# Attention on one core: the values of the global keys in four 64 x 64 parts of the array, guard and inverse of the sums ahead of the next step's masked blocks

## The chip, the cores and the metric

The kernel runs on one core of a Trainium2 chip. The metric is the device time of one execution in microseconds. A core has five engines with queues of their own: PE (TensorE, matrix products into the PSUM banks), DVE (VectorE), ACT (ScalarE), POOL (GpSimd) and SP (SyncE, here only for issuing DMAs). They are ordered against each other by semaphores alone.

## What is computed

An attention with 8 heads over 4 batches, with 32 global tokens and 512 local ones, followed by two parts with matmuls (a mix of each token with the one before it, then 8 experts with a gate). Only the attention is touched here:

```python
k_all = np.concatenate([k_g, k_l], axis=2)
v_all = np.concatenate([v_g, v_l], axis=2)
s_g = scale * np.matmul(q_g, k_all.transpose(0, 1, 3, 2))
out_g = np.matmul(sm(s_g), v_all)
s_ll = scale * np.matmul(q_l, k_l.transpose(0, 1, 3, 2))
mask = np.abs(pos[:, None] - pos[None, :]) <= window
s_ll = np.where(mask, s_ll, -1000000000.0)
s_lg = scale * np.matmul(q_l, k_g.transpose(0, 1, 3, 2))
a_l = sm(np.concatenate([s_lg, s_ll], axis=-1))
out_l = np.matmul(a_l, np.concatenate([v_g, v_l], axis=2))
```

`sm` subtracts the maximum, takes the exponential and divides by the sum plus 1e-9. A local token sees the 32 global keys and the local ones at most 32 away.

## The kernel before

The heads of a batch are worked on in two quads of four heads. A quad has five units: four of 128 local tokens each (`j` = 0 to 3) and one of the 32 global tokens (`j` is None). So a batch has `UNITS` = 10 units, the attention 40. Each engine has a `step(b, t)` for each unit, written out by hand, and semaphores keep the engines in step. A unit passes through the stages of a pipeline:

- PE, step t: `scores(t)` (L760 for a local unit, with 64 rows and 64 columns of the array, four parts in use; L774 for the global one, 128 rows and 64 columns) into `ps_s`.
- DVE, step t: `mask_scores(t)`: for each of the four heads one block of 160 columns (L1209: scale, mask, negative maximum) into `neg`. For the global unit one instruction (L1217).
- ACT, step t: `exponentials(t)`: for each head one exponential (L1800), with its sum, into `prob` and `rsum`.
- DVE, step t + 1: `guard_sums(t)` adds the 1e-9 (L1228) and `invert_sums(t)` takes the inverse (L1236).
- POOL, step t + 1: it copies the global keys' share of the probabilities (`edge`, L591) and spreads the inverse over 64 columns a head (`rb`, L602, L600 for the global unit), and then does half of a weight chunk of the next part: rounding (L576) or the rest (`lo` part, L580).
- PE, step t + 1: `turn(t)`: transposes of `prob` (L790, L800, and L794 to L796 for the global unit), of `edge` (L792) and of `rb` (L804), which alone waits for `spread`.
- DVE copies one half of the transposes to `probT` (`copy_turned`, L1244, semaphore `probT_b`), ACT the other (L1810, `probT_a`), both behind their other work of step t + 1.
- PE, step t + 2: `apply(t)`: products with the values, into `ps_o`: first the global keys (L827, values `vz`; for head k only rows 32 k to 32 k + 31 of `vz` are not zero), then the local ones (L836). For the global unit L851 to L858.
- DVE, step t + 2: `write_x(t)` (L1258) multiplies by the turned inverse and writes `xT`.

PE's order in a step is scores(t), apply(t - 2), turn(t - 1). DVE's is masked blocks of t, write_x(t - 2), copy_turned(t - 1), with guard and inverse of t - 1 behind the first and the second masked block. For a step with the global unit they stand ahead of everything:

```python
                last = behind(b, t, 1)
                if last and unit(t)[1] is None:
                    guard_sums(*last)
                    invert_sums(*last)
                mask_scores(b, t, last)
```

In the last batch DVE and ACT also do `first_inputs(t)` in each step: the first inputs of the next part (L1282, L1286 `mix_lo` on DVE, L1823, L1827 on ACT). Behind the attention PE goes on with `keys_part(0, GT, 0)`, which waits for those inputs and for POOL's last weight chunk; the last `apply` stands behind it.

SP loads the queries, keys and values of batch b into the same tiles when batch b - 1 has used them.

Of the kernel before, what the change touches and what calls it, by code (L numbers as in the profile page):

```python
# [34 lines left out]
P = 128  # L35
# [5 lines left out]
QB = P // 2  # L41
HALO = 2 * WIN + QB
KW = HALO + SG
HEADS = 4
# [118 lines left out]
def program(nc, qk_t, qg_t, v_t, v_x, v_z, mu, w_9, w_9t, w_mix, w_e, out, x2_d):  # L163
    with ExitStack() as ctx:
# [574 lines left out]
        def _(pe):  # L739
# [67 lines left out]
            def apply(b, t):  # L807
                i, j = unit(t)
                n = UNITS * b + t
                o = ps_o[:, t % 2, :]  # L810

# [9 lines left out]
                if j is not None:  # L821
                    pe.wait_ge(v_loaded[i][j], 16 * (b + 1))
                    if j == 0:
                        pe.wait_ge(vz_loaded[i], 16 * (b + 1))
                    for pair in range(2):
                        for h in range(2):
                            pe.matmul(o[DH * h:DH * (h + 1), P * pair:P * (pair + 1)], vz[i][:, 2 * pair + h, :],  # L827
                                      pt(HEADS), start=(pair == 0), stop=False)
                    for pair in (1, 0):
                        if pair == 0:  # L830
                            pe.wait_ge(probT_a, n + 1)
                        for blk in range(2):
                            for h in range(2):
                                k = 2 * pair + h
                                v0 = HEADS * DH * blk + DH * k
                                mm = pe.matmul(o[DH * h:DH * (h + 1), P * pair + QB * blk:P * pair + QB * (blk + 1)],  # L836
                                               vw[i][:, j, v0:v0 + DH], pt(k, QB * blk, QB), start=False, stop=(pair == 0 and blk == 1))
                else:
                    pe.wait_ge(vx_loaded[i], 16 * (b + 1))
                    rows = P - WIN  # L840
                    for cs in ((2, 3, 4), (0, 1)):
                        if cs[0] == 0:
                            pe.wait_ge(probT_a, n + 1)
                        for pair in range(2):
                            for c in cs:
                                for h in range(2):
                                    k = 2 * pair + h
                                    od = o[DH * h:DH * (h + 1), SG * pair:SG * (pair + 1)]
                                    v0 = HEADS * DH + DH * k
                                    if c < JT - 1:  # L850
                                        mm = pe.matmul(od, vw[i][:, c, v0:v0 + DH], pt(c, SG * k, SG),  # L851
                                                       start=(c == 2 and pair == 0),
                                                       stop=(c == 1 and pair == 1))
                                    elif c < JT:
                                        mm = pe.matmul(od, vw[i][0:rows, c, v0:v0 + DH], pt(c, SG * k, SG, rows),
                                                       start=False, stop=False)
                                    else:
                                        mm = pe.matmul(od, vx[i][:, DH * k:DH * (k + 1)], pt(c, SG * k, SG, rows),  # L858
                                                       start=False, stop=False)
# [326 lines left out]
        def _(dve):  # L1186
# [7 lines left out]

            def mask_scores(b, t, last):

# [8 lines left out]
                if j is not None:  # L1205
                    m = 0 if j == 0 else 2 if j == JT - 1 else 1
                    for k in range(HEADS):
# [3 lines left out]
                                                 negmax[:, t % 2, k:k + 1]).then_inc(masked, 1)  # L1211
                        if last and k == 0:
                            guard_sums(*last)
                        if last and k == 1:
                            invert_sums(*last)
                else:
# [29 lines left out]
            def write_x(b, t):  # L1246
                i, j = unit(t)
                o, sums = ps_o[:, t % 2, :], probT[:, t % 2, 2 * P:4 * P]
                x = xT[:, 2 * i:2 * i + 2, bass.ds(S * b + 1, SG) if j is None else bass.ds(S * b + 1 + SG + P * j, P)]
                dve.wait_ge(applied, UNITS * b + t + 1)  # L1250
                if j is None:
                    sums = sums[:, 0:P].rearrange("p (a h q) -> p a h q", a=2, h=2)
                    for h in range(2):
                        rows = slice(DH * h, DH * (h + 1))
                        ins = dve.tensor_tensor(x[rows], o[rows, 0:2 * SG].rearrange("p (a q) -> p a q", a=2),
                                                sums[rows, :, h, :], ALU.mult)
                else:
                    ins = dve.tensor_tensor(x, o[:, 0:2 * P].rearrange("p (a q) -> p a q", a=2),  # L1258
                                            sums.rearrange("p (a q) -> p a q", a=2), ALU.mult)
                ins.then_inc(x_written, 1)  # L1260

            def step(b, t):

                last = behind(b, t, 1)
                if last and unit(t)[1] is None:
                    guard_sums(*last)
                    invert_sums(*last)
                mask_scores(b, t, last)
                if behind(b, t, 2):
# [862 lines left out]
```

## Time and profile before

| | |
|---|---|
| median of 3 runs | 622.44 us (621.17 to 623.4) |
| profiled execution | 623.0 us, span 621.2 us |
| granted clock of PE over the span | 0.998 |
| PE busy | 607.2 us, 98% |
| DVE busy | 412.6 us, 66% |
| ACT busy | 321.5 us, 52% |
| POOL busy | 172.5 us, 28% |

The span runs from the first to the last instruction of the profiled execution; the difference to its time lies around it. Busy time counts instructions that work, not waiting. Matmuls are pipelined and their ends are modelled, so a busy PE is not one at its peak. PEld are the loads of the array's stationary operand, which overlap the matmuls. A 32-bit matmul shows as two records. The granted clock is the share of the full 2.4 GHz that PE was given.

### The profile page before, as it was taken

To read this page: it belongs to the slowest core of one execution; us is meant where nothing else is said; L and a number is where in the kernel's file an instruction comes from. 1 tells how busy PE (TensorE), PEld (TensorE's weight loads), DVE (VectorE), ACT (ScalarE), POOL (GpSimd) and SP (SyncE) were. 2 spreads that over 40 slices of the span, in tenths; PEclk is the share of its full clock that TensorE was granted. 3 is DMA by queue.
4 is the path that set the end of the run, shared out by engine and by line. 5 is a ranking of instruction groups with operands and counts; after the bars stand their busy time and mean duration, and the time that the engine had idled before them with its cause. 6 is when DMAs were issued, how large, how long until landed. Compare 5 with 4: busy or idle time off the path is not lost.

```text
span 621.2 us, 14687 instructions
## 1 busy us (share of the span) xinstructions
PE 607.2 (98%) x4483; PEld 504.5 (81%) x4484; DVE 412.6 (66%) x1164; ACT 321.5 (52%) x698; POOL 172.5 (28%) x241
## 2 busy tenths in 40 slices
PE   7989999999999999999999999999999999999996
PEld 6878888888888888889979878788788888888885
DVE  4767779845888797786979958957735335463541
ACT  5767779768516614632544844637526225362531
POOL 4545545600000000000000231285632521544141
PEclk9999999999999999999999999999999999999999
DMA  8987786002120010000004751886933512754000
GB/s 307 377 272 249 268 288 212 18 2 85 57 80 0 1 51 18 0 34 35 0 21 168 247 227 52 285 305 221 328 127 106 213 62 81 256 197 154 17 17 15
DMA packets 32935, 84.66 MB, mean 136 GB/s; under 512 B 4602, under 2 KB 7418, under 8 KB 32896
## 3 DMA queue, kind: packets, MB, share of 16 engines
q1 hardware_dynamic: 26816, 70.03, 32.5%
q0 software_dynamic: 3200, 8.92, 4.1%
q10 hardware_dynamic: 2880, 5.24, 2.6%
q8 instruction: 19, 0.31, 0.2%
q14 instruction: 20, 0.16, 0.1%
HBM read 76.04 MB, written 9.70 MB: 138 GB/s over the span
## 4 chain that ended last, share of the span: by engine, by line
PE 90%; DVE 6%; issue 2%; ACT 1%; POOL 1%; DVEq 0%; ACTq 0%; POOLq 0%
PE banks L889 23%; PE banks L891 23%; PE banks L890 23%; PE banks L760 3%; PE banks L1079 3%; PE banks L827 2%; DVE we_lo L1531 2%; PE banks L836 2%; PE banks L790 2%; PE banks L774 1%; PE banks L804 1%; PE banks L998 1%; PE banks L800 1%; PE banks L851 1%; DVE neg L1209 1%
## 5 line engine op out<-in xcount | busy, mean ns | idle before, releaser
L1498 DVE CUSTOM_DVE_ANT_0 product<-x,xT 128x512 f32<-128x512 f32 x120 | 77.8, 687 | 1.2 <-DMA xT<-in_w 1.2
L1800 ACT ACTIVATE prob<-neg,negmax 128x160 f32<-128x160 f32 (+1 forms) x136 | 59.1, 436 | 29.7 <-DVE negmax L1209 20.1
L1778 DVE TENSOR_SCALAR hid<-banks 128x512 f32<-128x512 f32 x34 | 23.5, 690 | 72.6 <-PE banks L891 71.5
L889 PE MATMUL banks<-we_hi,hid_hi 128*128 (+1 forms) x160 | 66.4, 415 | 1.6 <-DVE hid_lo L1611 1.6
L1910 ACT ACTIVATE k_sum<-banks 128x512 f32<-128x512 f32 (+2 forms) x40 | 21.4, 534 | 89.4 <-PE banks L891 84.7
L889 PE MATMUL banks<-we_hi,xg_hi 128*128 (+1 forms) x160 | 64.6, 404 | 1.3 <-DVE we_lo L1531 1.3
L891 PE MATMUL banks<-we_hi,xg_lo 128*128 (+1 forms) x160 | 62.6, 391 | 0.0
L891 PE MATMUL banks<-we_hi,hid_lo 128*128 (+1 forms) x160 | 62.6, 391 | 0.0
L890 PE MATMUL banks<-we_lo,hid_hi 128*128 (+1 forms) x160 | 62.6, 391 | 0.0
L890 PE MATMUL banks<-we_lo,xg_hi 128*128 (+1 forms) x160 | 62.4, 390 | 0.0
L686 POOL MEMSET xg<- 128x1024 f32 x1 | 1.0, 956 | 219.3 <-ACT k_raw L1903 219.3
L889 PE MATMUL banks<-mix_hi,wk_hi 128*128 128x512 f32 (+2 forms) x160 | 57.4, 358 | 0.2 <-POOL wr_lo L580 0.2
L891 PE MATMUL banks<-mix_hi,wk_lo 128*128 128x512 f32 (+2 forms) x160 | 57.1, 357 | 0.0
L890 PE MATMUL banks<-mix_lo,wk_hi 128*128 128x512 f32 (+2 forms) x160 | 57.1, 357 | 0.0
L1962 ACT ACTIVATE hid_hi<-banks 128x512 fp32r<-128x512 f32 x40 | 24.0, 600 | 60.8 <-PE banks L1079 60.7
L648 POOL TENSOR_TENSOR we_lo<-raw_end,we_hi 128x1024 f32 (+1 forms) x16 | 44.4, 2793 | 39.9 <-ACT we_hi L1890 29.8
L1209 DVE CUSTOM_DVE_ANT_0 neg<-banks,mask 128x160 f32<-128x160 f32 x128 | 37.7, 315 | 26.0 <-PE banks L760 24.7
L889 PE MATMUL banks<-wv_hi,k_hi 128*128 128x512 f32 x136 | 53.9, 396 | 0.0
L891 PE MATMUL banks<-wv_hi,k_lo 128*128 128x512 f32 x136 | 53.0, 390 | 0.0
L890 PE MATMUL banks<-wv_lo,k_hi 128*128 128x512 f32 x136 | 53.0, 389 | 0.0
L1611 DVE TENSOR_TENSOR hid_lo<-banks,hid_hi 128x512 fp32r<-128x512 f32 x40 | 27.6, 689 | 29.8 <-ACT hid_hi L1962 29.8
L1531 DVE TENSOR_TENSOR we_lo<-xT,we_hi 128x1024 f32 (+1 forms) x36 | 45.0, 1279 | 0.0
(295 smaller groups left out, 1465.0 us busy)
## 6 DMA issues: line engine op xcount, KB each, us to landing
xT<-in_w_e SPq DMA_DIRECT2D x36, 512.0 KB, 4.4
raw_end<-in_w_e SPq DMA_DIRECT2D x36, 512.0 KB, 4.9
qk<-in_qk_t SPq DMA_DIRECT2D x32, 448.0 KB, 6.3
vw<-in_v_t SPq DMA_DIRECT2D x32, 256.0 KB, 5.4
w_raw<-in_w_mix ACTq DMA_DIRECT2D x20, 256.0 KB, 4.1
x_rows<-x SPq DMA_DIRECT2D x17, 256.0 KB, 2.0
xT<-in_w SPq DMA_DIRECT2D x8, 256.0 KB, 3.4
vz<-in_v_z SPq DMA_DIRECT2D x8, 128.0 KB, 3.5
```

Of the source, the lines that this page charges most:

```text
L648: return pool.tensor_tensor(we_lo[:, buf, 2 * j:2 * j + 2, :].rearrange("p x a b -> p x (a b)"), raw_part(j).unsqueeze(1), we_hi[:, buf, 2 ...
L889: pe.matmul(dst, left[0], right[0], start=first, stop=False)
L890: pe.matmul(dst, left[0], right[1], start=False, stop=False)
L891: return pe.matmul(dst, left[1], right[0], start=False, stop=last)
L1209: dve.tensor_tensor_reduce(neg[:, KW * k:KW * (k + 1)], s[:, h, KW * pair:KW * (pair + 1)], mask[:, m, :], -SCALE, HUGE, ALU.add, ALU.min, ...
L1498: dve.tensor_tensor_reduce(product[:, k % 2, :], x2[:, t, :], w9(e), 1.0, 0.0, ALU.mult, ALU.add, dot[:, t % 2, e:e + 1]).then_inc(dotted, 1)
L1531: dve.tensor_tensor(we_lo[:, buf, 2 * j:2 * j + 2, :].rearrange("p x a b -> p x (a b)"), raw_part(j).unsqueeze(1), we_hi[:, buf, 2 * j:2 * ...
L1611: dve.tensor_tensor(hid_lo[:, D * h:D * (h + 1)], ps_ht[:, h, :], hid_hi[:, D * h:D * (h + 1)].bitcast(F32), ALU.subtract).then_inc(hid_lo ...
L1778: dve.tensor_scalar(hid[:, D * h:D * (h + 1)], ps_h[:, h, :], 0.0, None, ALU.max).then_inc(hid_ready, 1)
L1800: act.activation(prob[:, t % 2, c], neg[:, c], ACT.Exp, scale=-1.0, bias=negmax[:, t % 2, k:k + 1], accum_out=rsum[:, t % 2, k:k + 1]).the ...
L1910: act.activation(k_sum[:, f % 2, 0:w], ps_k[:, f % 2, 0:w], ACT.Relu).then_inc(k_copied, 1)
L1962: act.activation(hid_hi[:, D * h:D * (h + 1)], ps_ht[:, h, :], ACT.Copy).then_inc(hid_hi_ready, 1)
```

## The change

In `apply`, the products of the global keys' values use only the rows that are not zero for the pair of heads: rows 0 to 63 for the first pair, 64 to 127 for the second. With 64 columns for each head, the four matmuls of a unit lie in four parts of the array. Parts with different rows write to different banks, so the sums of a unit now lie in both banks of `ps_o`, one for each pair, in the half `t % 2`, where they had a bank of their own before. The flags that start and stop the sums follow. One semaphore increment is added behind the waits. In DVE's step, guard and inverse of the unit before stand ahead of the masked blocks in each step, not only in those of the global unit.

```diff
-                o = ps_o[:, t % 2, :]
+                o = ps_o[:, :, P * (t % 2):P * (t % 2 + 1)]
...
+                    pe.sem_inc(stepped, 1)
                     for pair in range(2):
+                        rows = slice(2 * SG * pair, 2 * SG * (pair + 1))
                         for h in range(2):
-                            pe.matmul(o[DH * h:DH * (h + 1), P * pair:P * (pair + 1)], vz[i][:, 2 * pair + h, :],
-                                      pt(HEADS), start=(pair == 0), stop=False)
+                            pe.matmul(o[DH * h:DH * (h + 1), pair, :], vz[i][rows, 2 * pair + h, :], pt(HEADS)[rows],
+                                      start=True, stop=False)
...
-                                mm = pe.matmul(o[DH * h:DH * (h + 1), P * pair + QB * blk:P * pair + QB * (blk + 1)],
-                                               vw[i][:, j, v0:v0 + DH], pt(k, QB * blk, QB), start=False, stop=(pair == 0 and blk == 1))
+                                mm = pe.matmul(o[DH * h:DH * (h + 1), pair, QB * blk:QB * (blk + 1)],
+                                               vw[i][:, j, v0:v0 + DH], pt(k, QB * blk, QB), start=False, stop=(blk == 1))
...
-            def mask_scores(b, t, last):
+            def mask_scores(b, t):
...
-                        if last and k == 0:
-                            guard_sums(*last)
-                        if last and k == 1:
-                            invert_sums(*last)
...
-                    ins = dve.tensor_tensor(x, o[:, 0:2 * P].rearrange("p (a q) -> p a q", a=2),
+                    ins = dve.tensor_tensor(x, o,
                                             sums.rearrange("p (a q) -> p a q", a=2), ALU.mult)
...
                 last = behind(b, t, 1)
-                if last and unit(t)[1] is None:
+                if last:
                     guard_sums(*last)
                     invert_sums(*last)
-                mask_scores(b, t, last)
+                mask_scores(b, t)
```

On DVE, in step 3 of the first batch, the queue of the kernel before reads from its first masked block's maximum on (L1228 is the guard, L1236 the inverse, L1209 a masked block and the reading of its maximum):

```order
L1209 ISA negmax 128x1
L1228 TENSOR_TENSOR rsum<-rsum,eps 128x4 [waits exped]
L1209 ISA neg,negmax<-banks,mask 128x160
L1209 ISA negmax 128x1
L1236 RECIPROCAL rinv<-rsum 128x4 [waits spread,summed]
L1209 ISA neg,negmax<-banks,mask 128x160
L1209 ISA negmax 128x1
```

In the changed kernel the same place reads as follows (L1233 is the inverse, L1210 a masked block):

```order
L1233 RECIPROCAL rinv<-rsum 128x4 [waits spread,summed]
L1210 ISA neg,negmax<-banks,mask 128x160 [waits scored,exped]
L1210 ISA negmax 128x1
L1210 ISA neg,negmax<-banks,mask 128x160
L1210 ISA negmax 128x1
L1210 ISA neg,negmax<-banks,mask 128x160
L1210 ISA negmax 128x1
```

The guard (L1225) stands directly ahead of this piece. Both instructions have moved ahead of the first masked block and of its wait for the scores; nothing else of DVE's order has moved.

On PE the order is that of before, here in the same step (L760 scores, L829 the products in question, L838 those with the local values, L790 the first transpose):

```order
L760 MATMUL banks<-qk 64x160 [waits quad0_qk3_loaded,masked]
L760 MATMUL banks<-qk 64x160 x7
L829 MATMUL banks<-probT,vz 64x128 [waits probT_b,quad0_v1_loaded]
L829 MATMUL banks<-probT,vz 64x128 x3
L838 MATMUL banks<-probT,vw 64x64 x4
L838 MATMUL banks<-probT,vw 64x64 [waits probT_a]
L838 MATMUL banks<-probT,vw 64x64 x3
L790 MATMUL banks<-ident,prob 128x128 [waits probT_b,probT_a,exped]
```

What changes on PE is the number of rows that an instruction uses and the bank that it writes, not its place.

## Rows read from the trace of the kernel before

**Rows 1.** The page: busy time of PE, and the chain that ended last, by engine.

```profile
PE 607.2 (98%) x4483; PEld 504.5 (81%) x4484; DVE 412.6 (66%) x1164; ACT 321.5 (52%) x698; POOL 172.5 (28%) x241
...
PE 90%; DVE 6%; issue 2%; ACT 1%; POOL 1%; DVEq 0%; ACTq 0%; POOLq 0%
```

**Rows 2.** By stretch: length, busy PE, PEld, DVE, ACT, POOL, clock, DMA share, GB/s.

```profile
15.60:30.30 14.70, 14.29 (x259) 11.83 (x258) 10.30 (x56) 10.37 (x41) 7.16 (x15) 1.00 1.05 376
30.30:46.50 16.20, 14.65 (x259) 11.91 (x259) 10.44 (x56) 10.35 (x41) 7.93 (x16) 1.00 0.83 276
...
60.48:74.52 14.04, 14.04 (x259) 11.83 (x258) 10.26 (x56) 10.32 (x41) 7.72 (x15) 1.00 0.82 279
...
102.76:118.00 15.24, 15.24 (x287) 13.17 (x288) 14.66 (x63) 14.38 (x50) 9.17 (x16) 1.00 0.12 43
```

**Rows 3.** Chain of waits from 60 to 76 us: start, length, piece.

```profile
61.78 0.47 PE banks L827 x8
...
63.41 0.22 PE banks L804 x2
63.62 0.70 PE banks L760 x16
...
66.19 0.70 PE banks L760 x16
...
69.16 0.70 PE banks L760 x16
69.86 0.59 PE banks L827 x8
70.45 0.47 PE banks L836 x16
70.92 0.37 PE banks L790 x2
...
71.61 0.27 PE banks L804 x2
71.88 0.70 PE banks L760 x16
```

**Rows 4.** Timeline from 60 to 72 us: start, length, engine, instruction.

```profile
60.02 1.28 POOL L580 TENSOR_TENSOR wv_lo<-w_raw,wv_hi 128x512 fp32r<-128x512 f32 x1
...
60.85 0.19 ACT L1800 ACTIVATION_READ_ACCUMULATOR prob<-neg,negmax 128x1 f32 x1
...
61.07 0.25 DVE L1228 TENSOR_TENSOR rsum<-rsum,eps 128x4 f32<-128x4 f32 x1 [0.21 <-ACT prob L1800]
...
61.35 0.18 DVE L1236 RECIPROCAL rinv<-rsum 128x4 f32<-128x4 f32 x1
...
67.64 0.43 ACT L1800 ACTIVATE prob<-neg,negmax 128x160 f32<-128x160 f32 x1 [0.34 <-DVE negmax L1209]
...
69.21 0.18 ACT L1800 ACTIVATION_READ_ACCUMULATOR prob<-neg,negmax 128x1 f32 x1
...
70.18 0.33 DVE L1209 CUSTOM_DVE_ANT_0 neg<-banks,mask 128x160 f32<-128x160 f32 x1 [0.74 <-PE banks L760]
...
70.61 0.43 ACT L1800 ACTIVATE prob<-neg,negmax 128x160 f32<-128x160 f32 x1 [0.75 <-DVE negmax L1209]
...
70.84 0.29 DVE L1209 CUSTOM_DVE_ANT_0 neg<-banks,mask 128x160 f32<-128x160 f32 x1
...
71.06 0.32 DVE L1209 CUSTOM_DVE_ANT_0 neg<-banks,mask 128x160 f32<-128x160 f32 x1
...
71.64 0.55 DVE L1244 COPY probT<-banks 128x384 f32<-128x384 f32 x1
```

**Rows 5.** Timeline in the last batch: POOL's and DVE's subtraction side by side.

```profile
99.40 1.28 POOL L580 TENSOR_TENSOR wv_lo<-w_raw,wv_hi 128x512 fp32r<-128x512 f32 x1
...
100.16 1.07 DVE L1286 TENSOR_TENSOR mix_lo<-first_raw,mix_hi 128x512 fp32r<-128x512 f32 x1
```

More of the change, by code:

```diff
@@ L847, in apply @@
                                     k = 2 * pair + h
-                                    od = o[DH * h:DH * (h + 1), SG * pair:SG * (pair + 1)]
+                                    od = o[DH * h:DH * (h + 1), pair, 0:SG]
                                     v0 = HEADS * DH + DH * k
@@ L851, in apply @@
                                         mm = pe.matmul(od, vw[i][:, c, v0:v0 + DH], pt(c, SG * k, SG),
-                                                       start=(c == 2 and pair == 0),
-                                                       stop=(c == 1 and pair == 1))
+                                                       start=(c == 2), stop=(c == 1))
                                     elif c < JT:
@@ L1247, in write_x @@
                 i, j = unit(t)
-                o, sums = ps_o[:, t % 2, :], probT[:, t % 2, 2 * P:4 * P]
+                o, sums = ps_o[:, :, P * (t % 2):P * (t % 2 + 1)], probT[:, t % 2, 2 * P:4 * P]
                 x = xT[:, 2 * i:2 * i + 2, bass.ds(S * b + 1, SG) if j is None else bass.ds(S * b + 1 + SG + P * j, P)]
@@ L1254, in write_x @@
                         rows = slice(DH * h, DH * (h + 1))
-                        ins = dve.tensor_tensor(x[rows], o[rows, 0:2 * SG].rearrange("p (a q) -> p a q", a=2),
+                        ins = dve.tensor_tensor(x[rows], o[rows, :, 0:SG],
                                                 sums[rows, :, h, :], ALU.mult)
                 else:
-                    ins = dve.tensor_tensor(x, o[:, 0:2 * P].rearrange("p (a q) -> p a q", a=2),
+                    ins = dve.tensor_tensor(x, o,
                                             sums.rearrange("p (a q) -> p a q", a=2), ALU.mult)
```

## The prediction

> **What bounds the kernel now.** I read the page first. Its busy row has PE at 98% of the span, and the chain that ended last is 90% PE [rows 1]. Busy PE in a modelled profile proves little, so I went on to what PE does and waits for around the change. Everything that the diff touches lies in the attention, the first fifth of the span; behind it stand matmuls that the diff doesn't touch and whose first one waits for the end of the attention, so a microsecond won or lost there moves the end by a microsecond. I therefore cut the attention into stretches of one quad (five steps) with the view of busy time by stretch [rows 2]. The reader is to see two stages. In the second quad of batch 1 PE is busy for all of 14.04 us while DVE has 10.26: PE alone sets the pace. In the last batch DVE and ACT also make the first inputs of the next part: in its second quad DVE has 14.66 of 15.24 us and ACT 14.38. There DVE is full and PE only keeps up. In the second quad of batch 0 the DMA engines are full (share 1.05), and the quad behind it takes 16.20 us with PE busy for 14.65.
>
> Next I read the chain of waits inside one PE-bound quad [rows 3]. A piece lasts from the end of the matmuls before it to its own end, so its length is the price of the group with whatever drain stands in front. Last, the timeline of DVE, ACT and POOL in the same quad [rows 4], for how much room there is beside PE.
>
> **The values of the global keys on PE.** The count stays: 4 instructions, 8 records, for each of the 32 local units. Before, each has 128 rows and 64 columns of the array, so two run side by side. Their group takes 0.47 us behind matmuls of the same shape (L774, 128 x 64) and 0.59 behind the scores L760, which use 64 x 64 parts [rows 3]: a change of shape costs 0.12. The change behind L836 gives a second reading of that price: L790 takes 0.37, where two transposes behind transposes of the same shape (L804) take 0.22, so 0.15. What four parts side by side do is seen in L760: 0.70 us less 0.15 of drain is 0.55 for 16 records of 160 columns, 0.21 ns for each record and column; L827 has 0.47 / (8 x 128) = 0.46 ns. Eight records of 128 columns at the rate of L760 take 0.22 us; I take 0.25, since short groups round up.
>
> Now the shapes. Behind local scores the new L829 needs no drain, but L838 behind it, still 128 x 64, does. The unit behind the global scores L774 gets both. So for three of four local units: 0.59 becomes 0.25, and the next group gains 0.15: **-0.19 us**. For the fourth: 0.47 becomes 0.25 + 0.12, the next gains 0.15: **+0.05**. One quad: -0.57 + 0.05 = -0.52.
>
> By TensorEngine Tiling of the Trainium skill, Key Properties, a change of tiling mode drains the array and a change of tile alone doesn't. The 0.12 and 0.15 above agree with it, and it is what speaks against this change: the added drain takes back most of what the four parts give.
>
> The additional semaphore increment in front and the same three waits cost nothing that I can see: L760 has the same form (an increment behind two waits), and its gap in front is no longer than the drain. Its cover was a drain, which L829 no longer has; without it the cost is bounded by 0.06 us a unit, the order of the shortest handover between engines in these rows, doubled (ACT's last sum ends at 61.04, the guard that waits for it begins at 61.07): 0 to 2 us over 32 units. I take 0, because the three waits are over long before in this stage and L760 still streams, and keep the rest for the range.
>
> The new place of the sums (one bank for each pair) changes nothing in time: DVE reads the same 256 elements per partition, and the next unit's matmuls stand behind the copy that DVE does after this reading.
>
> **Guard and inverse in front.** Embedded, they stretch the distance of masked blocks from 0.22 us (70.84 to 71.06) to 0.33 (half of 70.18 to 70.84), twice, so about 0.2 in all. In front of a step's first masked block they run one behind the other: the step with the global scores already has this form: guard at 61.07, inverse at 61.35, and the next instruction could start at about 61.45, 0.38 in all, or 0.28 when DVE is busy before them [rows 4]. They wait for the last exponential of the unit before, which DVE must await before the first block anyway.
>
> In the PE-bound stage this lies in idle time: exponentials end at 69.39, the first block waits for the scores until 70.18, 0.79 us. What it brings: the inverse, now behind the second block and so some 0.6 us behind the start of the first, ends before that start; POOL's spread starts at least 0.6 us earlier, and L804 no longer waits for it. Today that wait is 0.05 (0.27 against 0.22 [rows 3]) in two steps of five, **-0.10** a quad; with a PE that arrives 0.2 earlier and the old place it would be 0.25 in each, which is why the two edits are to be counted together. PE's sum for a quad: -0.62. (A quad of before is 2.57, 2.97, 2.72 and 2.72 us for the steps with local scores, and 3.06 for the one with global scores, the rest of 14.04.)
>
> **What stands next behind PE.** Three cycles get close. (1) Exponentials: four take 1.75 us (67.64 to 69.39), then 0.03 to the guard, 0.38, and 0.43 from first block to first exponential (70.18 to 70.61): 2.59 us a step. PE's own steps become 2.38, 2.97, 2.48, 2.48 and 3.11 (sum 13.4). Those below 2.59 fall short by 0.21 and 0.11, and the long ones behind give it back, so the average is not bound. (2) DVE's copy of the turned blocks ends at 72.19 (71.64 + 0.55), L827 of the next step starts at 72.58: 0.39 to spare. The change takes about 0.2 (shorter step) and 0.12 (no drain) and gives back 0.2 (blocks undisturbed): 0.3 is left, but less the 0.1 to 0.2 of cycle 1. (3) ACT's copy, behind its exponentials, has 0.3 to spare and loses about the same. I allow 0.1 a quad for waits of this kind: **-0.5** a quad.
>
> **The last batch.** Where DVE is full, PE's gain is worth nothing, and guard and inverse cost 0.28 in place of 0.17: +0.11 in six local steps, +0.7. Against it: POOL's subtraction of the weight chunk ends at 100.68, and the DVE subtraction that begins at 100.16 takes 1.07 us, 0.55 of them behind that end [rows 5]. So DVE was held for 0.5 by an operation that stands behind POOL's spread. With the inverse some 0.6 earlier that overlap goes, here and in two like places (0.1 to 0.5 each), -0.9. By SBUF — State Buffer of the Trainium skill, the summary for kernel authors, an instruction of the vector engine with two SBUF inputs and one of GpSimd that reads SBUF exclude each other; this row agrees. I take -0.2 for the batch, between +0.7 and -1.1.
>
> **The sum.** Batches 1 (second quad) and 2: 3 x -0.5 = -1.5. First quad of batch 1, with PE idle for 1.55 us of it: -0.4. Batch 0, with full DMA engines and only two or three units in its first quad: -0.6. Last batch -0.2. Together -2.7 us. The profiled execution took 623.0 (span 621.2), which would give 620.3; the median of the runs shown is 622.4, so the time predicted is 619.7.
>
> **Rivals.**
> - Hidden (the cycles of DVE and ACT eat the gain). For it: slack of only 0.3 in two of them, DVE full in the last batch. Against: ACT, the fuller of the two, has 10.32 of 14.04 us in the PE-bound quad. It would leave -0.1 a quad in six, and +0.0 to +0.7 in the last batch: about -0.5, 621.9.
> - Slower: the row halves don't overlap. The mechanism is at L829: if the four parts take 0.47 as now, a local unit gains 0.03, one behind L774 gains 0.27, less the 0.10: +0.26 a quad, some +2.0 over the attention, and the last batch's +0.7: 625.1. It decides from a group of about 0.38 us upward (0.26 + 0.09 a quad for the last batch, over four units). Against it stands L760, with halves, banks and order laid out alike.
> - POOL holds the guard. At 61.07 the guard lasts 0.25 to 61.32, just when POOL's subtraction (60.02 + 1.28) ends; embedded it would not meet it. If the same happened twice a quad at 0.26 us, it would undo the gain: 622.4. The lock named on the page above is this rule. Against: the spread that releases POOL comes earlier too, and its subtraction then ends about 2.1 us behind a guard, before the next at 2.4 to 2.6.
>
> **How the numbers follow.** A difference of 0.3% (1.9 us) is about what a measurement can tell here. Forecast 0.60, hidden 0.26, POOL 0.05, slower 0.09. The forecast's own spread runs from -1.6 to -4.5 (no waits, cheaper drains, all three holds gone), so some 0.05 of it falls within 0.3%: faster 0.55, same 0.36, slower 0.09. The range goes from 618.2 to 622.4, which takes in the hidden case and leaves out the slower one and the ends.
>
> **What would show it.** L829 in the chain 0.25 behind local scores, L838 0.6 instead of 0.47, L804 always 0.22; a quad of 13.4 to 13.6 us in place of 14.0; a second quad of the last batch within 0.4 of 15.2. I am wrong if L829 takes 0.4 or more, if waits for the copies appear in front of L829, or if the masked blocks begin 0.2 us and more behind the scores in most steps.

## The result: slower by a quarter of a per cent

| | before | after |
|---|---|---|
| median, 22 runs each | 622.14 us (619.89 to 625.06) | 623.58 us (619.53 to 624.52) |
| ratio to before | | 1.0025 (95% interval 1.0015 to 1.0035) |
| profiled execution | 623.0 us, span 621.2 us | 623.91 us, span 621.9 us |
| granted clock of PE over the span | 0.998 | 0.996 |

The forecast was 619.7 us with a range of 618.2 to 622.4. The time lies above the range and on the other side of before. The page of the changed kernel, busy row and chain by engine, answers to [rows 1]:

```profile
PE 606.8 (98%) x4483; PEld 501.0 (81%) x4484; DVE 415.4 (67%) x1164; ACT 321.8 (52%) x698; POOL 176.4 (28%) x241
...
PE 84%; DVE 7%; issue 3%; ACT 2%; POOLq 1%; DMA 1%; POOL 1%; DVEq 0%; ACTq 0%
```

PE's busy time is the same within 0.4 us and its share of the chain fell from 90% to 84%: more of the end hangs on waits, but the page doesn't say where. So I cut the attention into quads, from the start of one L774 to the start of the next. The view by stretch of the changed kernel (columns as in [rows 2]) for the second quad of batch 0, the first of batch 1, the first of batch 2 and the last:

```profile
15.84:34.67 18.83, 15.44 (x259) 12.36 (x258) 11.32 (x57) 10.82 (x42) 7.97 (x14) 0.91 0.90 321
34.67:49.23 14.56, 14.03 (x259) 11.31 (x258) 10.73 (x56) 9.96 (x39) 7.41 (x15) 1.00 0.84 275
62.83:76.53 13.70, 13.64 (x259) 11.11 (x259) 10.96 (x57) 10.35 (x41) 7.54 (x15) 1.00 0.91 300
104.15:118.57 14.42, 13.99 (x259) 11.27 (x259) 14.06 (x61) 13.20 (x45) 8.09 (x14) 1.00 0.14 40
```

In the third of these rows PE is busy nearly throughout, and the quad is shorter than before; the quads in front of it and behind it are like it (table). The first row has PE idle for 3.4 us and a granted clock of 0.91. The last has DVE at 14.06 of 14.42 us. The table holds the same cut for both kernels, worked out from the starts of L774 in the two traces, in us:

| stretch | before | after | difference | forecast |
|---|---|---|---|---|
| up to the first L774 | 15.58 | 15.84 | +0.3 | |
| batch 0, second quad | 14.76 | 18.83 | +4.1 | |
| batch 1, first quad | 16.16 | 14.56 | -1.6 | |
| these three together | 46.50 | 49.23 | +2.7 | -1.0 |
| batch 1 second, batch 2 both | 13.98, 14.05, 13.98 | 13.60, 13.70, 13.59 | -1.1 | -1.5 |
| batch 3, first and second | 14.25, 13.89 | 14.03, 14.42 | +0.3 | -0.2 |
| attention to the next part's first matmul | 122.18 | 124.14 | +2.0 | -2.7 |

What lies behind the attention took 499.0 us in the profiled execution of before and 497.5 to 498.1 in those of all other kernels of this study, the changed one too. That execution of before was 0.9 above its median, and its surplus lay there, so only the attention is compared from here on.

**The PE-bound quads.** The chain of waits of the changed kernel (start, length, piece) answers to [rows 3]:

```profile
64.13 0.38 PE banks L829 x8
64.50 0.62 PE banks L838 x16
...
65.82 0.22 PE banks L804 x2
...
66.74 0.34 PE banks L829 x8
67.08 0.62 PE banks L838 x16
...
72.11 0.06 issue
72.17 0.45 PE banks L829 x8
...
74.15 0.70 PE banks L760 x16
74.85 0.22 PE banks L829 x8
75.07 0.62 PE banks L838 x16
```

L829 takes 0.22 us behind local scores when nothing holds it (74.85), 0.38 behind L774, and the drain has moved to L838 (0.62). L804 is 0.22 each time. But twice L829 is longer, 0.34 and 0.45. The two PE-bound quads beside this one have two longer pieces each as well, here in batch 1:

```profile
58.39 0.34 PE banks L829 x8
...
60.97 0.31 PE banks L829 x8
61.28 0.70 PE banks L838 x16
```

The timeline shows what holds L829 there. DVE's copy of the turned blocks ends at 58.14, and the first load of L829 begins 0.12 us later:

```profile
57.58 0.56 DVE L1241 COPY probT<-banks 128x384 f32<-128x384 f32 x1
58.26 0.24 PEld L829 LDWEIGHTS banks<-probT,vz 64*64 64x64 f32 x8 [0.16 <-issue]
```

It is 0.12 in all four long pieces of those two quads, so L829 waits for this copy. In the quad shown first it is not so: there the copies end 0.41 and 0.31 us ahead of L829's first load. These are the first local step of the loop's second pass and the first one with the batch's new values; what holds L829 in them is not shown.

**Batch 0.** The timeline of PE in the changed kernel (start, length, line; in brackets the idle time in front and what ended it):

```profile
25.11 0.78 PE L760 MATMUL banks<-qk 64*64 64x160 f32 x16
25.70 0.40 PE L829 MATMUL banks<-probT,vz 64*64 64x128 f32 x6
28.83 0.38 PE L829 MATMUL banks<-probT,vz 64*64 64x128 f32 x2 [2.73 <-issue]
29.14 0.69 PE L838 MATMUL banks<-probT,vw 128*64 128x64 f32 x16
```

PE stops in the middle of a group, behind the sixth of its eight records, where no wait stands in the program, for 2.73 us. Nothing in the profile released it: "issue" is time in which it waited for nothing that the profile shows. The same view of before:

```profile
25.08 0.66 PE L827 MATMUL banks<-probT,vz 128*64 128x128 f32 x8
26.14 0.69 PE L836 MATMUL banks<-probT,vw 128*64 128x64 f32 x16 [0.41 <-issue]
```

The same kind of stop, at nearly the same place, 0.41 us long. The views by stretch up to the stop, of the changed kernel and then of before, give the count of records in front of it: 339 + 341 = 680 and 341 + 342 = 683.

```profile
0.00:28.80 28.80, 22.38 (x339) 17.63 (x341) 15.58 (x87) 17.59 (x67) 13.79 (x35) 1.00 0.96 338
```

```profile
0.00:26.10 26.10, 22.37 (x341) 18.00 (x342) 14.02 (x84) 16.19 (x60) 12.62 (x33) 1.00 0.96 334
```

More stops of this kind, of 0.2 to 0.74 us, stand in before at 19.18, 34.02 and 41.34 us, with 248 and 249 records from one to the next and 237 up to the last, and in the changed kernel at 20.13 and 44.16. A stop at a fixed count of PE's records, with no semaphore behind it, looks like code that has not arrived. The view of the DMA queues bears it out: for 0.25 us from 26.00 in the changed kernel, and from 23.25 in before (packets, MB, share of 16 engines):

```profile
q1 hardware_dynamic: 30, 0.09, 95.5%
q8 instruction: 1, 0.02, 29.7%
```

```profile
q1 hardware_dynamic: 19, 0.06, 60.0%
q10 hardware_dynamic: 19, 0.04, 41.2%
q8 instruction: 1, 0.02, 25.9%
```

One packet of 16 KB on queue q8, kind "instruction", amid data that nearly fill the 16 engines. It starts at 26.05 in the changed kernel and at 23.47 in before, 2.8 and 2.7 us before PE resumes (28.83, 26.14). This distance holds everywhere: from 14 to 62 us the 18 profiles of this study have 29 stops of PE over 0.3 us that nothing released, and each ends 2.3 to 2.8 us after such a packet starts. In the changed kernel the packet starts just as PE comes to its stop (28.83 - 2.73 = 26.10), 2.6 us later than in before, so almost its whole way is paid for.

Whose packets are they? PE runs batch 0 as straight-line code and batches 1 to 3 as three passes of one loop. The packets of q8 come every 4 to 11 us up to the end of the loop's first pass (the last at 61.30 in before, 63.52 in the changed kernel), and none comes in any profile from 67 to 118 us, in the passes that repeat the same code. The view of the queues of before from 66 to 118 us has instruction packets of q14 alone:

```profile
q1 hardware_dynamic: 4375, 8.62, 49.4%
q10 hardware_dynamic: 1296, 2.36, 14.2%
q14 instruction: 5, 0.04, 0.2%
```

The stop has a second price. By stretches of 2 us in the changed kernel (last three columns: granted clock, DMA share, GB/s):

```profile
26.00:28.00 2.00, 0.10 (x3) 0.00 (x0) 1.15 (x9) 1.59 (x8) 0.99 (x3) 1.00 1.04 369
28.00:30.00 2.00, 1.17 (x20) 0.93 (x20) 0.13 (x1) 0.30 (x2) 0.00 (x0) 0.98 1.04 380
30.00:32.00 2.00, 2.00 (x19) 1.63 (x21) 1.10 (x4) 0.58 (x1) 0.82 (x3) 0.50 0.88 307
32.00:34.00 2.00, 2.00 (x38) 1.56 (x31) 1.08 (x9) 0.66 (x4) 1.11 (x1) 0.67 0.19 67
```

Behind a pause of nearly 3 us the granted clock is 0.50 from 30 to 32 us, which is 1.2 GHz, and 0.67 from 32 to 34, a mean of both levels. PE is busy for all of these 4 us and does 0.50 and 0.67 of a stretch's work: 1.0 + 0.66 = 1.7 us lost. Some comes back: the DMA share has fallen to 0.19 by 32 us, PE is idle for 0.53 us in the first quad of batch 1 and not for 1.55, and that quad is 1.6 us shorter than before.

The single profile is no exception. Each execution has its mean granted clock on record: in 19 of the 22 of the changed kernel it is 0.997 or less, and in 3 of 35 of before (those beside runs 1 to 4). But a stop of this length need not cost the clock. Run 3 below has the same stop, 2.46 us long, and stays at 1.00 behind it:

```profile
30.00:32.00 2.00, 2.00 (x46) 1.63 (x44) 1.40 (x7) 0.62 (x2) 1.21 (x3) 1.00 0.92 316
```

### The profile page after: what moved, and what is told of

It reads as the page before. It is cut to its first block, busy times and chain, and to the rows that moved or that the text cites. A ratio compares the mean times of both kernels' runs of the same rounds, so it can differ in the third digit from the quotient of the medians.

```text
span 621.9 us, 14714 instructions
## 1 busy us (share of the span) xinstructions
PE 606.8 (98%) x4483; PEld 501.0 (81%) x4484; DVE 415.4 (67%) x1164; ACT 321.8 (52%) x698; POOL 176.4 (28%) x241
## 4 chain that ended last, share of the span: by engine, by line
PE 84%; DVE 7%; issue 3%; ACT 2%; POOLq 1%; DMA 1%; POOL 1%; DVEq 0%; ACTq 0%
PE banks L890 22%; PE banks L892 22%; PE banks L891 22%; PE banks L760 3%; PE banks L1080 3%; PE banks L838 2%; DVE we_lo L1528 2%; PE banks L790 1%; PE banks L829 1%; PE banks L999 1%; DVE neg L1210 1%; PE banks L774 1%; PE banks L800 1%; POOLq L724 1%; DMA xg<-x_rows,rows_in 1%
## 5 line engine op out<-in xcount | busy, mean ns | idle before, releaser
L1528 DVE TENSOR_TENSOR we_lo<-xT,we_hi 128x1024 f32 (+1 forms) x36 | 42.9, 1220 | 0.0
L1210 DVE CUSTOM_DVE_ANT_0 neg<-banks,mask 128x160 f32<-128x160 f32 x128 | 34.0, 321 | 13.3 <-PE banks L760 11.7
```

What stands on the lines that cost most here:

```text
L1210: dve.tensor_tensor_reduce(neg[:, KW * k:KW * (k + 1)], s[:, h, KW * pair:KW * (pair + 1)], mask[:, m, :], -SCALE, HUGE, ALU.add, ALU.min, ...
L1528: dve.tensor_tensor(we_lo[:, buf, 2 * j:2 * j + 2, :].rearrange("p x a b -> p x (a b)"), raw_part(j).unsqueeze(1), we_hi[:, buf, 2 * j:2 * ...
```

## The experiments

Three theories: **the increments** in PE's straight-line code of batch 0 make its code arrive later among full-length loads; guard and inverse in front cost in **the last batch**; **the four parts** bring less than counted. (The letters in the recorded expectations are their own: in runs 1 to 3 A is the last batch and B the increment with the loads of code, in 5 and 6 C is the length of PE's code.) The attention's length is that of one profiled execution each, which can lie some us off its median.

**1. The four parts alone.** The changed kernel with guard and inverse between the masked blocks, as before:

```diff
...
-                if last:
+                if last and unit(t)[1] is None:
```

> The four parts alone; guard and inverse stay between the masked blocks. Theory A (the last batch pays for guard and inverse in front, and batch 0 loses time in stalls that have nothing to do with them): the PE-bound quads take 13.75 to 13.85 us in place of 14.0, since the last transposes now wait 0.2 us longer for the spread inverse; the last batch is back at 28.1 us between its first and last global scores; the whole is 0 to 1.5 us faster than before. Theory B (the edit in front is harmless and the four parts cost the time, through the increment and the loads of code in batch 0): no faster than before, +1 to +2 us like the full change.

Measured: 623.97 us, ratio 1.0036 (1.0023 to 1.0049), attention 125.65. The long stop is there (PE resumes at 28.41), and the PE-bound quads are 13.97, 14.11 and 13.98: no gain at all, where 13.75 to 13.85 was expected. The chain of waits shows why:

```profile
73.21 0.37 PE banks L829 x8
73.58 0.62 PE banks L838 x16
...
74.89 0.34 PE banks L804 x2
```

L829 is held (0.37 instead of 0.22), and L804, which waits for the spread of the inverse, is 0.34 instead of 0.22. So the place where this edit is worth anything is made by the other one.

**2. Guard and inverse in front alone**, added to before (the reverse of that line in before):

> Guard and inverse in front alone, products of the global values as before. Theory A: PE-bound quads gain the 0.1 us of the wait for the spread inverse at most (13.9), the last batch gets longer by 0.3 to 0.9 us, the whole is 0 to +1 us against before. Theory B: no change at all (within 0.5 us).

Measured: 620.69 us, ratio 0.9980 (0.9968 to 0.9991), attention 120.87. PE-bound quads 13.89, 13.89, 13.88: -0.1 each, as forecast. The last quad is 14.41 (13.89 before). So half of the change is a gain by itself, and neither theory of the expectation had that. Most of it doesn't come from what the edit does in a PE-bound quad: in this profile the three stops of before (0.41, 0.64 and 0.74 us) are gone or under 0.3, and the second quad of batch 0 and the first of batch 1 take 14.37 and 13.88 us instead of 14.76 and 16.16. Run 12 has the same edit, but for the last batch, where such stops hardly cost anything.

**3. Guard and inverse in front, but not in the last batch.**

```diff
+            def front(b, t):
+                return unit(t)[1] is None or not (isinstance(b, int) and b == B - 1)
...
```

> The full change, but in the last batch, where DVE is full, guard and inverse stay between the masked blocks. Theory A: the last batch gives back what it lost, so the time falls below that of the full change by 0.3 to 0.9 us. Theory B: as the full change, +1.5 us against before.

Measured: 623.06 us, ratio 1.0025 (1.0011 to 1.0039), attention 123.47. The last quad is back at 13.94, the one ahead of it goes from 14.03 to 14.31: 0.2 us between them, less than the medians can tell. The price in the last batch is real in its place and too small to be the cause.

**4. The changed kernel without the increments in batch 0.**

```diff
-                    pe.sem_inc(stepped, 1)
+                    if not first_batch(b):
+                        pe.sem_inc(stepped, 1)
```

> The full change, but the added increment stands only in the loop over batches 1 to 3, not in the eight local units of batch 0, so that the code of PE in batch 0 is as long as before. If the 3 us gap inside L829 of batch 0 (6 of 8 records, then 2.7 us of nothing) is a late load of code whose place follows the length of the code, it moves or shrinks and the time falls by 1 to 3 us. If it is a matter of when the other loads run, the gap stays and the time is that of the full change.

Measured: 621.28 us, ratio 0.9990 (0.9977 to 1.0004), attention 121.37. Eight increments fewer are worth 1.0025 - 0.9990 = 0.0035, or 2.2 us. PE resumes at 26.88 instead of 28.83 and keeps its clock; the packet on the instruction queue comes at 24.25 to 24.50:

```profile
25.16 0.40 PE L830 MATMUL banks<-probT,vz 64*64 64x128 f32 x8
26.88 0.69 PE L839 MATMUL banks<-probT,vw 128*64 128x64 f32 x16 [1.33 <-issue]
```

**5. Before with the eight increments.** The added increment, in before, in batch 0 alone.

> The kernel before, with nothing but the eight increments that the change puts in front of L827 in batch 0. Theory C (the length of PE's code in batch 0 decides when a block of code is asked for, and that load then stands behind the loads of keys and queries): the 16 KB load of code that ran at 23.3 us before runs at about 26, PE stands still for 1.5 to 3 us inside the group of L827 in the second quad, and the time is +1 to +2 us against before. Theory D (the increments don't matter; the faster products themselves move PE so that the load comes late): no change, within 0.5 us.

Measured: 622.38 us, ratio 1.0009 (0.9998 to 1.0019), attention 121.72; the packet starts at 24.50 (23.47 before), PE resumes at 27.11 (26.14). But the first L774 stands 0.57 us later too, and the stop is as long as before (0.42 and 0.41 us). So the +1 to +2 us that theory C of the expectation asked for don't appear, and the interval doesn't tell the ratio from 1: the increments cost what they do only together with the rest of the change.

**6. Batch 1's first keys loaded later.** Their load waits for eight scored units in place of five:

```diff
-                    sp.wait_ge(scored, UNITS * (b - 1) + 5 * i + 5)
+                    sp.wait_ge(scored, 8 if b == 1 and i == 0 else UNITS * (b - 1) + 5 * i + 5)
```

> The full change, but SP issues the keys and queries of batch 1's first quad after eight units are scored and not after five. Theory C: the load of code no longer stands behind them, it runs at 22 to 24 us as before the change or earlier, the gap inside L829 shrinks from 2.7 us to less than 1, and the time falls by 1 to 2.5 us against the full change, unless the later loads make batch 1 wait at its start (they need some 8 us and have about 7). If the code load is late for a reason of its own, it stays at 26 us.

Measured: 623.39 us, ratio 1.0025 (1.0010 to 1.0039), attention 124.11. The stop of batch 0 goes (second quad 13.40), its packet comes at 21.68. Another one follows behind the postponed burst, 2.26 us long at 42.80, and the first quad of batch 1 is 17.58. The stall goes where the burst goes, and nothing is won. (In this profile the first L774 is late as well, at 18.19: PE waited 1.58 us for values at 12.29, and the granted clock was 0.50 for 3.4 us behind that.)

**7. Edits 3 and 4 together.**

> The full change with increments only in the loop and with guard and inverse between the masked blocks in the last batch: 0.2 us less than the run with the increments in the loop alone (which stood at 0.999 of before), so 0.998 to 0.999.

Measured: 620.11 us, ratio 0.9977 (0.9961 to 0.9993), attention 124.18, twelve runs from 618.69 to 624.22. The profiled execution is the slowest of them and shows what the longer ones can have: a stop of 2.83 us before 42.03, with the granted clock at 0.50 from 41.3 to 48.2 us.

```profile
26.19 0.69 PE L839 MATMUL banks<-probT,vw 128*64 128x64 f32 x16 [0.72 <-issue]
42.03 0.81 PE L760 MATMUL banks<-qk 64*64 64x160 f32 x8 [2.83 <-issue]
```

**8. Before with the front in batches 0 to 2 only.**

> The kernel before with guard and inverse in front in batches 0 to 2 alone. The edit in front alone stood at 0.998; the last batch should give back 0.2 us: 0.9975 to 0.998, the best of all versions so far.

Measured: 620.69 us, ratio 0.9981 (0.9967 to 0.9994), attention 119.80: the same as run 2. Leaving out the last batch changes nothing that can be told.

**9 to 12. Loads paced.** SP issues the keys of one unit each time one more unit is scored, and its values when one more is applied, in place of a whole quad at once; the bytes are the same. Added to the changed kernel (9), before (10), run 7 (11) and run 8 (12):

```diff
-                    sp.wait_ge(scored, UNITS * (b - 1) + 5 * i + 5)
-                    load_scores(b, i)
-
-                    sp.wait_ge(applied, UNITS * (b - 1) + 5 * i + 5)
-                    load_values(b, i)
+                    done = UNITS * (b - 1) + 5 * i + 5
...
+                    for j in range(JT):
+                        sp.wait_ge(scored, done + j)
+                        sp.dma_start(qk[i][:, j, :], qk_t[rows + P * j:rows + P * (j + 1)]).then_inc(qk_loaded[i][j], 16)
+                        sp.wait_ge(applied, done + j)
...
+                        sp.dma_start(vw[i][:, j, :], v_t[rows + P * j:rows + P * (j + 1)]).then_inc(v_loaded[i][j], 16)
```

> The full change, with the same loads for batches 1 to 3 issued one by one: SP issues the keys and queries of a unit, and then its values, when one more unit is scored and applied, and not all four of a quad at once. Theory C' (a load of PE's code that is asked for behind four queued loads comes late, and that costs what the change wins): no gap over 1 us in PE's batches 0 and 1, the granted clock stays at 1.00, both quads there take 13.5 to 14 us, and the time falls to 0.995 to 0.998 of before. If the stalls have another cause they stay, and the time is that of the full change (1.0025).

> The kernel before with the paced loads. Theory C': it too loses its stalls (0.5, 1.0 and 0.9 us in batches 0 and 1), so 0.996 to 0.998; the distance to the full change with paced loads is then what the change wins in the attention itself, 1 to 2 us. Otherwise: 1.000.

> Increments only in the loop, guard and inverse embedded in the last batch, paced loads: 0.2 us less than the full change with paced loads; 0.994 to 0.997 of before, and no second cluster of runs 3 us higher as without the pacing.

> Guard and inverse in front in batches 0 to 2, products of the global values as before, paced loads: between the kernel before and the mended change with the same loads. If the four parts are worth what the PE-bound quads show (13.6 against 13.88 us), it is 1 to 2 us slower than the mended change with paced loads.

| | median, us | ratio to before | attention in the profile, us |
|---|---|---|---|
| 9, changed kernel | 619.11 | 0.9952 (0.9939 to 0.9966) | 120.33 |
| 10, before | 619.68 | 0.9963 (0.9949 to 0.9976) | 119.74 |
| 11, run 7 | 618.95 | 0.9951 (0.9937 to 0.9964) | 119.64 |
| 12, run 8 | 619.33 | 0.9961 (0.9947 to 0.9974) | 119.45 |

Pacing takes 4.5 us off the changed kernel and 2.4 off before. In the profiles of 10 and 12 no stop of PE over 0.3 us is left between 14 and 62 us; 11 has one of 0.64. That of 9, the longest of its five runs, still has one of 1.91 us in batch 0, where none over 1 was expected, but the clock stays up behind it:

```profile
30.00:32.00 2.00, 2.00 (x35) 1.73 (x33) 1.86 (x10) 1.43 (x7) 1.33 (x2) 1.00 0.98 320
```

Between 9 and 10 the change is worth 0.6 us on this ground, not the 1 to 2 expected; their intervals overlap, so its sign there is likely, not shown. Guard and inverse in front alone (12 against 10) are worth 0.0002, nothing that can be told, where they were 0.0019 with the loads in bursts (run 8). And 12 is 0.4 us slower than 11, not the 1 to 2 expected. So most of what the edits won or lost by themselves was a matter of where the stops fell.

**13 and 14. Length of PE's code.** `BETWEEN`, the warm-up matmuls in front of batch 0's first masked step, from 6 to 2 in the changed kernel, and to 10 in run 4:

> The full change with its eight increments in batch 0, but four of the six idle transposes behind the second scores are left out (eight instructions of PE fewer, all ahead of the place). If the length of the code up to a point decides when its blocks are asked for, the stalls are those of the run with the increments in the loop alone: 0.999 of before. If it is the increments themselves, 1.0025 stays.

> The reverse: increments in the loop alone (0.999), with four idle transposes more. By the length of the code this is as slow as the full change, 1.002 to 1.003, with the code load at about 26 us and a gap of more than 2 us behind it; if it is the increments themselves, 0.999.

Measured: 622.88 us, ratio 1.0029 (1.0008 to 1.0049), attention 123.52, and 621.30 us, ratio 1.0003 (0.9990 to 1.0016), attention 120.18. By the length of the code it would have been the other way round. In 13 PE stops before 28.61, with the count of records at that stop unchanged:

```profile
0.00:28.00 28.00, 20.75 (x339) 16.81 (x341) 15.46 (x87) 17.32 (x66) 13.73 (x35) 1.00 0.96 338
```

With four matmuls fewer ahead of it the stop stands four records later in the program (behind the second record of L838, not the sixth of L829), and four earlier in 14 than in 4. So a block of code ends at a fixed count of PE's instructions. But moving that end did not help 13: its packet comes at 25.96, as late as the changed kernel's, and PE stops for 2.19 us; in 14 it comes at 23.20 and PE stops for 0.47. That the increments cost time because they push PE's code past the end of a block is ruled out. What sets the length of the stop is when the packet comes.

**16. The increments ahead of the waits.** Run 4 with the eight increments of batch 0 put back, but in front of L829's waits:

```diff
+                if j is not None and first_batch(b):
+                    pe.sem_inc(stepped, 1)
                 pe.wait_ge(probT_b, n + 1)
...
```

> The full change, but in batch 0 the eight increments stand ahead of the waits of the product's group and not behind them. If an increment behind waits holds PE's reading of its code until the waits are over, and the next block is therefore asked for later, this is as fast as the run with the increments in the loop alone (0.999 to 1.000), with the code load at 23 to 24.5 us. If eight increments cost this wherever they stand, 1.0025 and a code load at 26 us.

Measured: 621.76 us, ratio 1.0003 (0.9988 to 1.0018), attention 123.26; the packet comes at 24.16 (26.05 behind the waits, 24.42 without increments). Going by the ratios, the increments cost 0.0013 (0.8 us) ahead of the waits, which these intervals don't tell from nothing, and 0.0035 (2.2 us) behind them. Their place behind the waits seems to be most of it; the intervals of this run and of the changed kernel just touch. The packets say the same: with the loads in bursts at their old place it starts at 25.76 to 26.08 us in the four profiles with the four parts and increments behind waits (changed kernel, runs 1, 3, 13), and at 23.20 to 24.42 in the four without them or with them ahead (runs 4, 7, 14, 16).

**15. The best of these.** Run 11, with guard and inverse in front also in the first quad of the last batch:

```diff
...
+                return unit(t)[1] is None or not (isinstance(b, int) and b == B - 1 and t >= 5)
...
```

> Increments in the loop, paced loads, guard and inverse in front but for the second quad of the last batch. In the profiles the first quad of that batch takes 14.04 us with them in front and 14.3 embedded, the second 14.40 and 13.95. So 0.25 us less than the mended change with paced loads, 0.9945 to 0.995 of before.

Measured: 618.52 us (seven runs, 617.19 to 620.26), ratio 0.9952 (0.9934 to 0.9970), attention 118.86. It is the fastest median, but not to be told from runs 9 to 12.

## Why the prediction was wrong

**The step that failed** is the one on batch 0 and the first quad of batch 1: "Batch 0, with full DMA engines and only two or three units in its first quad: -0.6", "First quad of batch 1, with PE idle for 1.55 us of it: -0.4". They took +2.7 us: the stop for code grew from 0.41 to 2.73 us (+2.3), and the clock behind it cost 1.7, of which the first quad of batch 1 gave some back. I had both signs in [rows 2], the DMA share of 1.05 and the 1.55 us in which PE was idle, and scaled the gain down for them instead of asking what ended that idle time. The answer stood in the timeline of before: "issue", not a semaphore. In this stretch PE doesn't run on its own order and semaphores alone: its code comes through the same full DMA engines.

**The increments.** "The additional semaphore increment in front and the same three waits cost nothing that I can see", with a bound of 0 to 2 us. Run 4 puts 2.2 us on the eight of batch 0 alone, outside that bound. The bound was from the wrong resource, the shortest handover between engines; the cost came with a later packet of code. L760, on which I leaned, has its increment behind waits too, and it was there before.

**The four parts.** The mechanism was right. L829 behind local scores is 0.22 (I took 0.25), behind L774 0.38 (0.37), L838 0.62 (0.62). The rival of halves that don't overlap is excluded. The size was off: -0.35 to -0.39 a quad, not -0.5, guard and inverse included. I had written "I allow 0.1 a quad for waits of this kind". With the pieces as measured PE's own sum is -0.70 (L829 at 0.22 and not 0.25), so the waits took 0.3 to 0.35 a quad. In two of the three quads most of that is the wait for DVE's copy, which I had given 0.3 us of room. The rest of the forecast's size was off too: with paced loads, where fewer stops are left, the whole change is worth 0.6 us (9 against 10), not 2.7.

**Guard and inverse in front** brought -0.1 in a PE-bound quad (run 2), as forecast. That they are "to be counted together" with the four parts holds more strongly than I put it: alone the parts bring nothing in these quads (run 1).

**The last batch**, forecast -0.2, was +0.3: the first quad -0.2, the second +0.5. The holds did go, as forecast; the view of one tile gives shortest, median and longest of DVE's subtraction L1283, first of the changed kernel, then of before (L1286):

```profile
L1283 DVE TENSOR_TENSOR mix_lo<-first_raw,mix_hi x4: 684/688/745, 101.9 to 119.3; 128x512 fp32r<-128x512 f32 x4
```

```profile
L1286 DVE TENSOR_TENSOR mix_lo<-first_raw,mix_hi x4: 680/932/1072, 100.2 to 116.9; 128x512 fp32r<-128x512 f32 x4
```

What failed is the price of guard and inverse where DVE is full, "0.28 in place of 0.17". The timeline of DVE and POOL in the changed kernel:

```profile
113.66 0.65 POOL L591 COPY edge<-prob 128x128 f32<-128x128 f32 x1 [0.57 <-ACT prob L1797]
...
114.08 0.25 DVE L1225 TENSOR_TENSOR rsum<-rsum,eps 128x4 f32<-128x4 f32 x1
114.37 0.18 DVE L1233 RECIPROCAL rinv<-rsum 128x4 f32<-128x4 f32 x1
114.57 0.32 DVE L1210 CUSTOM_DVE_ANT_0 neg<-banks,mask 128x160 f32<-128x160 f32 x1
```

From the guard's start to the first masked block it is 0.49 us, and 0.48 or 0.49 in all five steps from 99 us on in which the guard takes four sums. Between the blocks, before, the pair cost 0.15: the four blocks of a step start within 0.88 us with it ([rows 4], 70.18 to 71.06) and within 0.73 or 0.74 without; my 0.17 (0.2 where I worked it out) was near that. So six steps cost about +1.9 us on DVE, not +0.7. The vanished holds paid 0.8 of it, as forecast (-0.9): the four subtractions take 2.81 us in place of 3.62. What took up the rest, down to the +0.3 measured, is not shown.

The guard lasts 0.25 here, with POOL's copy of the edge beside it, and ends when the copy ends (114.31). Where that copy starts just behind the guard, it lasts 0.16 (at 72.02). From 100 to 119 us its mean is 233 ns here and 169 in before. By the rule of SBUF — State Buffer of the Trainium skill (summary for kernel authors), a vector instruction with two SBUF inputs and one of GpSimd that reads SBUF exclude each other, and the guard's inputs are both in SBUF; the 0.25 against 0.16 us agree with it. So the rival "POOL holds the guard" was right in kind, but with another operation of POOL than the one that I named, and with 0.09 us a time and not 0.26. It isn't the whole price either: at 72.02, where the guard isn't held, the first block follows after 0.49 as well.

**What stays open.** No view names the packet's owner. That it brings PE's code is read from three things: the stop has no releaser and stands in the middle of a group, it ends 2.3 to 2.8 us after a packet of q8 starts, and these packets are absent while PE repeats its loop. That an increment behind waits delays the packet is shown by runs 4 and 16 in packets, and by run 4 in times; how it does so (whether PE's sequencer reads no further ahead until the waits are over) was only argued. Why the same line costs 0.6 us in before (run 5, an interval that holds 1) and 2.2 in the changed kernel isn't settled either, and the four parts alone without the increments were not run. When the clock falls behind a stop isn't settled: it fell behind stops of 1.47 us (run 16, at 41.57), 2.19 (run 13), 2.54 (run 1) and 2.73, and not behind 1.91 (run 9) and 2.46 (run 3).

## What to carry to other kernels

Where PE is idle without a releaser ("issue") beside a DMA share near 1, look for packets on the instruction queue before costing anything in that stretch: a small edit there moves a stall, and a stall can cost the clock as well. Try spreading loads over the steps rather than issuing them in one burst; here that took 2.4 us off the kernel before and 4.5 off the changed one. When two edits feed one wait, run each alone: half of this change was a gain by itself (0.9980), the other half, with its increments, a loss (1.0036). And repeat such runs with the stalls out of the way, because the gain of the one half was gone there (0.9961 against 0.9963).

## What the runs showed of the hardware

- Packets of 16 KB on one instruction queue went through the same 16 DMA engines as data, while PE ran straight-line code or a loop's first pass, and none in the loop's later passes. PE's stops stood 248 or 249 of its records apart in straight-line code and ended 2.3 to 2.8 us after such a packet started (29 stops over 0.3 us in 18 profiles, the longest 2.83 us). With the same bytes paced none over 0.3 us was left in runs 10 and 12, one each of 0.64 and 1.34 in 11 and 15, and two of 0.38 and 1.91 in 9.
- After a stop of 2.73 us the granted clock was 0.50 for 2 us and 0.67 in the mean of the next 2. After one of 1.47 (run 16) it fell to 0.50 too; after 1.91 (run 9) and 2.46 (run 3) it stayed at 1.00.
- Eight records of 128 columns in four 64 x 64 parts took 0.22 us, against 0.47 in two parts of 128 x 64; a change of shape cost 0.12 to 0.16.
- Two short DVE instructions of which the second needs the first took 0.49 us in a row up to the start of the next instruction, with a copy on POOL beside them, and added 0.15 between independent ones.
